# MLP blocks of 512 and 384 tokens in place of 448, in an attention and mixing kernel on one core

## The chip, the cores and the metric

The kernel runs on one core of a Trainium2 chip. The metric is the device time of one execution in microseconds. Before the change it is 916.15 us, the median of three runs (915.28 to 916.17). The profiled execution is a fourth one, 912.93 us long.

## What is computed

Batch 4, 12 heads of 64, so 768 features; 448 tokens per batch. Three stages follow each other:

```python
scores = cap * tanh((q @ k.T / 8) / cap)          # attention, per head
x = softmax(scores) @ v                           # -> (4, 448, 768)
theta = x @ w_theta                               # first mixer
y = w_tok_r @ (x * cos(theta)) + w_tok_i @ (x * sin(theta))
u = x + y
x = u + relu(u @ w_ch)
u = x + (relu(x.T @ w_tok1) @ w_tok2).T           # second mixer, over tokens
out = u + relu(u @ w_ch1) @ w_ch2                 # MLP, 768 -> 1536 -> 768
```

The last line is the MLP. It mixes features only, so any cut of the 4 x 448 tokens into blocks gives the same result.

## The kernel before

Everything is kept transposed: features on the 128 partitions, in six tiles (`D_TILES`), tokens along the free dimension. Each product of two fp32 matrices is made of three fp32r matmuls (`products`, lines 1036 to 1038): high part by high part, high by low, low by high. So every operand is split into a `hi` part (a copy that rounds, mostly on ScalarE) and a `lo` part (value minus `hi`, mostly on VectorE).

Memory: `x_t` holds the activations of all four batches, batch after batch, 6 x 448 floats of each partition per batch. The attention writes it pair of heads by pair, the first mixer adds to it, the token mixer writes it again, and the MLP adds its result in place.

Order of the work after the attention: the angles and token products of the first mixer for four batches, written out; then `token_mix(b)` for four batches; then the MLP, `rise_and_fall(b)` on TensorE. Each engine has its own program, the order in it is as written, and semaphores tie the engines together. `loop_peeled` writes the first and the last batch out and makes a hardware loop of the two in the middle: on TensorE for both stages, on ScalarE and VectorE for `token_mix`.

The MLP of one batch: `up(b, c)` multiplies one of 12 tiles of `w_ch1` by `u` (6 feature tiles x 3 products = 18 matmuls of 448 columns) into PSUM bank 0 or 1; ScalarE makes `relu_hi` of it (L757) and VectorE `relu_lo` (L1020); `down(b, c)` multiplies the tile of `w_ch2` by these (6 output tiles x 3 products = 18 matmuls) and adds up in the banks 2 to 7 over the 12 tiles. TensorE's order is up(1), down(0), up(2), down(1), ..., up(11), down(10), down(11). So `down(10)` and `down(11)`, 36 matmuls, lie between the last `up` of a batch and the first `up` of the next one. In that time ScalarE makes `relu_hi` of tile 11 and then `u_hi` of the next batch (L742), and VectorE makes `u_lo` of it (L928); `up` of the next batch waits for `u_lo_made`. After that VectorE adds the banks 2 to 7 to `x_t` (L1029), and SyncE stores the result in two halves (L512).

`up(0, 0)` comes early, inside `token_mix(3)`, in the place in which the other batches have `channel(b + 1, 0)`: after `tokens_up(b, 1)`. It too waits for `u_lo_made`.

The activations of batches 2 and 3 are written to memory before the MLP (`spill`, L492), since the weights of tile 11 and two of the three `relu` buffers lie in their place; they are read back into the place of batches 0 and 1 as soon as the outputs of these are stored (L517).

Of the kernel before, what the change touches and what calls it, by code (L numbers as in the profile page):

```python
# [19 lines left out]
F32 = mybir.dt.float32  # L20
# [7 lines left out]
P = 128  # L28
# [8 lines left out]
BANK = 512  # L37
HEAD_TILES = SEQ // P
# [27 lines left out]
def mixer_kernel(nc, kq_t, v, cap, w_theta, w_tok_r_t, w_tok_i_t, w_ch, w_tok1, w_tok2,  # L66
                 w_ch1, w_ch2, out_t, sum_scratch, inverse_scratch, u_scratch):
    ctx = ExitStack()
    with ctx:
# [14 lines left out]
        x_t = place("x_t", [P, BATCH * D_TILES * SEQ], F32, AT_X)  # L84

        def x_tile(b, d, n=1):

            return x_t[:, bass.ds((b * D_TILES + d) * SEQ, n * SEQ)]
# [104 lines left out]
        o += 21504  # L193
# [24 lines left out]
        ring_at = [o, AT_X + X_BYTES // 2 + 12288, AT_X + X_BYTES // 2 + 12288 + 3584]  # L218
        relu_hi = [place(f"relu_hi{s}", [P, SEQ], F32R, at) for s, at in enumerate(ring_at)]
        relu_lo = [place(f"relu_lo{s}", [P, SEQ], F32R, at + 1792) for s, at in enumerate(ring_at)]  # L220
        assert o + 3584 <= AT_TOP
# [103 lines left out]
        def after(engine, semaphore, value):  # L325

            if not isinstance(value, int) or value > 0:
                engine.wait_ge(semaphore, value)

        def loop_peeled(engine, n, body):  # L330

            body(0)
            with engine.Fori(1, n - 1) as i:
                body(i)
            body(n - 1)

# [32 lines left out]
        def _(sp):  # L371
# [48 lines left out]
            def copy_x(b):  # L420

                after(sp, x_rows_ready, BEFORE[b])
                x_b = x_tile(b, 0, D_TILES).rearrange("p (d n) -> p d n", n=SEQ)
                sp.dma_start(x_batch[:, :, 0:SEQ], x_b).then_inc(x_copied, 16)
                if b % 2 == 0:
                    next_b = x_tile(b + 1, 0, D_TILES).rearrange("p (d n) -> p d n", n=SEQ)
# [61 lines left out]

            def spill(b):

                sp.wait_ge(u2_made, D_TILES * (b + 1))
                sp.dma_start(u_scratch[b - 2].rearrange("(d p) n -> p d n", p=P),  # L492
                             x_t[:, b * D_TILES * SEQ:(b + 1) * D_TILES * SEQ].rearrange(
                                 "p (d n) -> p d n", n=SEQ)).then_inc(spilled, 16)
# [13 lines left out]
            for b in range(BATCH):  # L508
                for half in range(2):
                    d0 = 3 * half  # L510
                    sp.wait_ge(out_made, D_TILES * b + d0 + 3)
                    sp.dma_start(out_t[b, d0 * P:(d0 + 3) * P, :].rearrange("(d p) n -> p d n", p=P),  # L512
                                 x_t[:, ((b % 2) * D_TILES + d0) * SEQ:((b % 2) * D_TILES + d0 + 3) * SEQ
                                     ].rearrange("p (d n) -> p d n", n=SEQ)).then_inc(out_stored, 16)
# [841 lines left out]
```

## Time and profile before

| | |
|---|---|
| profiled execution | 912.93 us |
| its span, first to last instruction | 910.9 us |
| TensorE busy | 893.6 us, 98% of the span |
| VectorE, ScalarE, GpSimd busy | 438.4, 305.9, 191.0 us |
| mean DMA rate | 62 GB/s |
| stages: attention; first mixer; token mix; MLP | 0 to 182; 182 to 387; 387 to 553; 546 to 911 us |

The busy time of TensorE is that of overlapping matmuls, whose ends are modelled: 368 ns are given for one of 448 columns, though the next starts 207 ns later. The distance from start to start is what a matmul costs. `PE` is TensorE, `PEld` its weight loads, `DVE` VectorE, `ACT` ScalarE, `SP` SyncE. In the chain of waits matmuls of the MLP alone (lines 1036 to 1038) are the largest part.

### The profile page before, as it was taken

The numbers are of one execution on the slowest core, as the hardware profiler recorded it, in microseconds if no ns is written. First come the engines' busy times: TensorE is split into PE (matmuls) and PEld (weight loads), VectorE is DVE, ScalarE is ACT, GpSimd is POOL, SyncE is SP. The second block draws the span as 40 slices with busy tenths as digits, with TensorE's granted clock in tenths as the row PEclk, the third lists the DMA queues.
The fourth block names the chain that finished last, engine by engine and source line by source line (L and its number), as shares of the span: only waits on it lengthen the run. The fifth ranks groups of instructions, "written<-read, shape, count | busy, mean of one in ns | idle before, by whom it ended". The sixth has DMA issues, their size and how long they took to land.

```text
span 910.9 us, 12549 instructions
## 1 busy us (share of the span) xinstructions
PE 893.6 (98%) x5248; PEld 754.9 (83%) x5248; DVE 438.4 (48%) x593; ACT 305.9 (34%) x355; POOL 191.0 (21%) x139
## 2 busy tenths in 40 slices
PE   8999999998999999999999999999999999999998
PEld 5445444597999889999999999999999999999997
DVE  5899998798584968724243442223200310031002
ACT  6999998645151434412122121112000100010000
POOL 0245545247050533270000024600000000000000
PEclk9999999999999999999999999999999999999999
DMA  6555764412020200230000136200300030000001
GB/s 160 163 135 150 181 171 114 124 43 61 1 70 1 62 1 27 78 110 1 1 0 0 61 104 217 87 1 1 122 1 0 1 121 0 0 25 37 1 1 61
DMA packets 40514, 56.76 MB, mean 62 GB/s; under 512 B 5744, under 2 KB 36624, under 8 KB 40464
## 3 DMA queue, kind: packets, MB, share of 16 engines
q1 hardware_dynamic: 40240, 55.82, 21.0%
q8 instruction: 37, 0.61, 0.3%
q10 hardware_dynamic: 224, 0.23, 0.1%
q14 instruction: 13, 0.11, 0.0%
HBM read 41.62 MB, written 8.52 MB: 55 GB/s over the span
## 4 chain that ended last, share of the span: by engine, by line
PE 87%; DVE 8%; issue 2%; ACT 1%; POOL 1%; DMA 0%; DVEq 0%; ACTq 0%
PE psum L1036 23%; PE psum L1038 23%; PE psum L1037 23%; PE psum L1078 8%; PE psum L1048 5%; PE psum L1053 2%; PE psum L1105 2%; DVE sin_z L897 2%; PE psum L1201 1%; DVE reduced L890 1%; DVE reduced L886 1%; DVE tile_sums L790 1%; PE psum L1151 1%; DVE tail_z L914 0%; DMA kq_raw<-kq_t 0%
## 5 line engine op out<-in xcount | busy, mean ns | idle before, releaser
L1020 DVE SCALAR_TENSOR_TENSOR relu_lo<-psum,relu_hi 128x448 fp32r<-128x448 f32 x48 | 30.0, 625 | 280.5 <-PE psum L1038 263.6
L757 ACT ACTIVATE relu_hi<-psum 128x448 fp32r<-128x448 f32 x48 | 26.2, 546 | 312.7 <-PE psum L1038 303.0
L1037 PE MATMUL psum<-relu_lo,mlp 128*128 128x448 f32 x288 | 106.1, 368 | 0.0
L1038 PE MATMUL psum<-relu_hi,mlp 128*128 128x448 f32 x288 | 106.1, 368 | 0.0
L1038 PE MATMUL psum<-u_hi,mlp 128*128 128x448 f32 x288 | 106.1, 368 | 0.0
L1036 PE MATMUL psum<-relu_hi,mlp 128*128 128x448 f32 x288 | 106.1, 368 | 0.0
L1037 PE MATMUL psum<-u_lo,mlp 128*128 128x448 f32 x288 | 106.1, 368 | 0.0
L1036 PE MATMUL psum<-u_hi,mlp 128*128 128x448 f32 x288 | 106.0, 368 | 0.0
L1078 PE MATMUL psum<-ring,values 128*32 128x448 f32 x768 | 82.5, 549 | 1.2 <-issue 1.2
L631 ACT ACTIVATE ring<-psum,score_scale 128x1792 f32<-128x1792 f32 (+1 forms) x48 | 75.3, 1568 | 17.9 <-PE psum L1105 10.0
L634 ACT ACTIVATE ring<-ring,cap_col 128x1792 f32<-128x1792 f32 (+1 forms) x48 | 77.1, 1606 | 1.6
L1078 PEld LDWEIGHTS psum<-ring,values 128*32 128x32 f32 x768 | 23.1, 111 | 45.3 <-issue 45.1
L1036 PE MATMUL psum<-theta_hi,x_hi 128*128 128x384 f32 x168 | 58.7, 349 | 0.0
L1036 PEld LDWEIGHTS psum<-relu_hi,mlp 128*128 128x128 f32 x288 | 54.1, 188 | 5.4
L1038 PEld LDWEIGHTS psum<-relu_hi,mlp 128*128 128x128 f32 x288 | 54.1, 188 | 5.4
L1037 PEld LDWEIGHTS psum<-relu_lo,mlp 128*128 128x128 f32 x288 | 54.1, 188 | 5.4
L1036 PEld LDWEIGHTS psum<-u_hi,mlp 128*128 128x128 f32 x288 | 54.1, 188 | 5.4
L1038 PEld LDWEIGHTS psum<-u_hi,mlp 128*128 128x128 f32 x288 | 54.1, 188 | 5.4
L1037 PEld LDWEIGHTS psum<-u_lo,mlp 128*128 128x128 f32 x288 | 54.1, 188 | 5.3
L1037 PE MATMUL psum<-theta_lo,x_hi 128*128 128x384 f32 x168 | 56.5, 336 | 0.0
L1038 PE MATMUL psum<-theta_hi,x_lo 128*128 128x384 f32 x168 | 56.5, 336 | 0.0
L1036 PE MATMUL psum<-u_hi,channel_hi 128*128 128x448 f32 x144 | 54.1, 375 | 0.0
(134 smaller groups left out, 1971.7 us busy)
## 6 DMA issues: line engine op xcount, KB each, us to landing
kq_raw<-kq_t SPq DMA_DIRECT2D x47, 224.0 KB, 3.8
mlp_raw<-moe_w_ch SPq DMA_DIRECT2D x24, 384.0 KB, 6.6
values<-v SPq DMA_DIRECT2D x48, 112.0 KB, 3.4
inverse_rows<-inverse_scratch SPq DMA_DIRECT2D x12, 448.0 KB, 6.0
x_batch<-x_t SPq DMA_DIRECT2D x4, 1344.0 KB, 6.4
out_t<-x_t SPq DMA_DIRECT2D x8, 672.0 KB, 3.1
u_scratch<-x_t SPq DMA_DIRECT2D x2, 1344.0 KB, 5.3
x_t<-u_scratch SPq DMA_DIRECT2D x2, 1344.0 KB, 5.8
```

The lines of the kernel that those rows point to most:

```text
L631: act.activation(places, psum[:, first:end, 0:SEQ], ACT.Tanh, scale=score_scale[:, :]).then_inc(tanh_done, 1)
L634: act.activation(places, places, ACT.Exp, scale=cap_col[:, :]).then_inc(probs_ready, 1)
L757: act.activation(relu_hi[c % 3][:, :], psum[:, c % 2, 0:SEQ], ACT.Relu).then_inc(relu_hi_made, 1)
L897: dve.tensor_scalar(sin_z[slot_of(b, m)][:, :], reduced[:, :], PI_BELOW, -PI_BELOW, ALU.min, ALU.max).then_inc(angles_ready, 1)
L1020: dve.scalar_tensor_tensor(out=relu_lo[c % 3][:, :], in0=psum[:, c % 2, 0:SEQ], scalar=0.0, in1=relu_hi[c % 3][:, :].bitcast(F32), op0=ALU ...
L1036: pe.matmul(out, left[0], right[0], start=start, stop=False)
L1037: pe.matmul(out, left[0], right[1], start=False, stop=False)
L1038: return pe.matmul(out, left[1], right[0], start=False, stop=stop)
L1048: b_mm = pe.matmul(psum[:, b_tile, 0:SEQ], left[s][b_rows, b_keys], right[s][b_rows, queries], start=step == 0, stop=step == 2 and b_tile ...
L1053: a_mm = pe.matmul(psum[:, a_tile, 0:SEQ], left[s][a_rows, a_keys], right[s][a_rows, queries], start=step == 0 and a_tile != T, stop=step ...
L1078: mm = pe.matmul(psum[rows, VALUES_BANK, 0:SEQ], own[:, block, 32 * h:32 * h + 32], ring[:, ring_place(pair, tile), :], start=n == 0, stop ...
L1105: mm = pe.matmul(psum[32 * n:32 * n + 32, SUMS_BANK, 0:SEQ], weights[:, :], moving, start=True, stop=True)
```

## The change

- The MLP goes over four blocks of tokens, `BLOCKS`: tokens 0 to 512 and 512 to 896 of batches 0 and 1 taken together, and the same of batches 2 and 3. Block 0 holds batch 0 and 64 tokens of batch 1.
- `x_t` is laid out as [half of two batches, feature tile, 896 tokens], so that a block is one strided view of it. A batch is now six rows of 448 with 896 between their starts.
- `u_hi` and `u_lo` of the MLP become `wide_hi` and `wide_lo`, with 512 places per feature tile; the `relu` buffers get 512 places. What lies behind them moves up by 3,072 bytes.
- A block's output is stored per half of the features and per batch: four DMAs for a block of 512 (448 and 64 tokens, twice), two for one of 384.
- The loops over batches are written out on all engines.

The diff, cut:

```diff
+BLOCKS = ((0, BANK), (BANK, 2 * SEQ)) * 2
...
-        x_t = place("x_t", [P, BATCH * D_TILES * SEQ], F32, AT_X)
+        x_t = place("x_t", [P, 2, D_TILES, 2 * SEQ], F32, AT_X)
+        def x_tile(b, d):
+            return x_t[:, b // 2, d, b % 2 * SEQ:(b % 2 + 1) * SEQ]
+        def x_of(b):
+            return x_t[:, b // 2, :, b % 2 * SEQ:(b % 2 + 1) * SEQ]
+        def x_block(k):
+            first, end = BLOCKS[k]
+            return x_t[:, 0, :, first:end]
...
-        o += 21504
+        wide_hi = place("wide_hi", [P, D_TILES, BANK], F32R, o)
+        wide_lo = place("wide_lo", [P, D_TILES, BANK], F32R, o + 12288)
+        o += 24576
...
+            for k, (first, end) in enumerate(BLOCKS):
                 for half in range(2):
                     d0 = 3 * half
+                    sp.wait_ge(out_made, D_TILES * k + d0 + 3)
+                    for b in range(2):
+                        n0, n1 = max(first, b * SEQ), min(end, (b + 1) * SEQ)
+                        if n0 < n1:
+                            sp.dma_start(out_t[k // 2 * 2 + b, d0 * P:(d0 + 3) * P, n0 - b * SEQ:n1 - b * SEQ
...
+                if k < 2:
+                    sp.wait_ge(out_stored, stored)
+                    sp.dma_start(x_block(k), spilled_rows[:, :, first:end]).then_inc(u_reloaded[k], 16)
...
-                if isinstance(b, int) and b == BATCH - 1:
-                    act.wait_ge(u2_made, D_TILES)
-                    make_u_hi(0)
+                if b == BATCH - 1:
+                    act.wait_ge(u2_made, D_TILES * 2)
+                    make_wide_hi(0)
...
-                    act.activation(relu_hi[c % 3][:, :], psum[:, c % 2, 0:SEQ], ACT.Relu
+                    act.activation(relu_hi[c % 3][:, 0:n_tokens], psum[:, c % 2, 0:n_tokens], ACT.Relu
...
+            def make_wide_lo(k):
+                tokens = slice(0, BLOCKS[k][1] - BLOCKS[k][0])
+                dve.wait_ge(u_hi_made, BATCH + k + 1)
+                dve.tensor_tensor(wide_lo[:, :, tokens], x_block(k), wide_hi[:, :, tokens].bitcast(F32),
+                                  ALU.subtract).then_inc(u_lo_made, 1)
...
-                    mm = products(psum[:, c % 2, 0:SEQ], (mlp[c][:, 0, part], mlp[c][:, 1, part]),
-                                  (u_hi[:, k, :], u_lo[:, k, :]), k == 0, k == D_TILES - 1)
+                    mm = products(psum[:, c % 2, tokens], (mlp[c][:, 0, part], mlp[c][:, 1, part]),
+                                  (wide_hi[:, d, tokens], wide_lo[:, d, tokens]), d == 0, d == D_TILES - 1)
...
-            loop_peeled(pe, BATCH, rise_and_fall)
+            for k in range(len(BLOCKS)):
+                rise_and_fall(k)
```

The order of the instructions stays the same outside the loops; what changes is their size, block by block. On ScalarE, from the last `relu_hi` of the second batch of the MLP to the third (before; the number behind a name is that of the buffer):

```order
L757 ACTIVATE relu_hi_151<-psum 128x448
L757 ACTIVATE relu_hi_152<-psum 128x448
L742 ACTIVATE u_hi<-x_t 128x2688
L757 ACTIVATE relu_hi_150<-psum 128x448
L757 ACTIVATE relu_hi_151<-psum 128x448
```

The same place now, between the second block and the third:

```order
L761 ACTIVATE relu_hi_153<-psum 128x384
L761 ACTIVATE relu_hi_154<-psum 128x384
L697 ACTIVATE wide_hi<-x_t 128x3072
L761 ACTIVATE relu_hi_152<-psum 128x512
L761 ACTIVATE relu_hi_153<-psum 128x512
```

The copy between the blocks has 3,072 elements per partition instead of 2,688, and it stands behind a block of 384 columns. On VectorE, the end of `token_mix(3)` before (`u_lo` is what `up(0, 0)` waits for, the first and third row add the token mixer's result):

```order
L982 TENSOR_TENSOR x_t<-psum,block_t 128x448
L928 TENSOR_TENSOR u_lo<-x_t,u_hi 128x2688
L982 TENSOR_TENSOR x_t<-psum,block_t 128x448
L976 SCALAR_TENSOR_TENSOR hidden_lo<-psum,hidden_hi 128x384 x2
L982 TENSOR_TENSOR x_t<-psum,block_t 128x448 x3
L1020 SCALAR_TENSOR_TENSOR relu_lo_153<-psum,relu_hi_150 128x448
```

And now:

```order
L990 TENSOR_TENSOR x_t<-psum,block_t 128x448
L936 TENSOR_TENSOR wide_lo<-x_t,wide_hi 128x3072
L990 TENSOR_TENSOR x_t<-psum,block_t 128x448
L984 SCALAR_TENSOR_TENSOR hidden_lo<-psum,hidden_hi 128x384 x2
L990 TENSOR_TENSOR x_t<-psum,block_t 128x448 x3
L1032 SCALAR_TENSOR_TENSOR relu_lo_155<-psum,relu_hi_152 128x512
```

Nothing moved there but the size of the subtraction, 2,688 to 3,072.

## Rows read from the trace of the kernel before

**Rows 1.** The page: busy time and share of the span of each engine.

```profile
PE 893.6 (98%) x5248; PEld 754.9 (83%) x5248; DVE 438.4 (48%) x593; ACT 305.9 (34%) x355; POOL 191.0 (21%) x139
```

**Rows 2.** Stretches, TensorE: length, busy (matmuls), granted clock, DMA share, GB/s.

```profile
638.80:728.06 89.26, 89.26 (x434) 1.00 0.09 31
728.06:817.32 89.26, 89.26 (x434) 1.00 0.09 31
240.74:243.69 2.95, 2.95 (x19) 1.00 0.00 0
262.15:266.42 4.27, 4.27 (x22) 1.00 0.60 164
```

**Rows 3.** Timeline, TensorE, token mix: start us, length us, line, tiles, shape.

```profile
419.63 0.34 PE L1036 MATMUL psum<-rows_hi,tok_hi 112*128 112x384 f32 x1
423.88 0.37 PE L1036 MATMUL psum<-u_hi,channel_hi 128*128 128x448 f32 x1
464.56 0.37 PE L1036 MATMUL psum<-u_hi,channel_hi 128*128 128x448 f32 x1
505.25 0.37 PE L1036 MATMUL psum<-u_hi,channel_hi 128*128 128x448 f32 x1
545.94 0.36 PE L1036 MATMUL psum<-u_hi,mlp 128*128 128x448 f32 x1
```

**Rows 4.** Timeline, TensorE, first mixer: angle products (384), token products (448).

```profile
240.91 0.34 PE L1038 MATMUL psum<-theta_hi,x_lo 128*128 128x384 f32 x1
243.51 0.34 PE L1038 MATMUL psum<-theta_hi,x_lo 128*128 128x384 f32 x1
262.15 0.36 PE L1036 MATMUL psum<-token_hi,tail_hi 128*128 128x448 f32 x1
266.42 0.37 PE L1036 MATMUL psum<-token_hi,tail_hi 128*128 128x448 f32 x1
```

**Rows 5.** Timeline around `up(0, 0)`: ScalarE, VectorE, weight loads (PEld).

```profile
539.93 2.44 ACT L691 ACTIVATE u_hi<-x_t 128x2688 fp32r<-128x2688 f32 x1
542.41 3.02 DVE L928 TENSOR_TENSOR u_lo<-x_t,u_hi 128x2688 fp32r<-128x2688 f32 x1 [1.11 <-ACT u_hi L691]
545.76 0.19 PEld L1036 LDWEIGHTS psum<-u_hi,mlp 128*128 128x128 f32 x1
```

**Rows 6.** Timeline between the second and the third batch of the MLP.

```profile
720.82 0.55 ACT L757 ACTIVATE relu_hi<-psum 128x448 fp32r<-128x448 f32 x1 [6.89 <-PE psum L1038]
721.26 2.44 ACT L742 ACTIVATE u_hi<-x_t 128x2688 fp32r<-128x2688 f32 x1
723.73 2.96 DVE L928 TENSOR_TENSOR u_lo<-x_t,u_hi 128x2688 fp32r<-128x2688 f32 x1 [1.71 <-ACT u_hi L742]
727.85 0.19 PEld L1036 LDWEIGHTS psum<-u_hi,mlp 128*128 128x128 f32 x1
```

**Rows 7.** Single lines: durations min/median/max in ns, first and last start.

```profile
L645 ACT ACTIVATE x_hi<-x_t x1: 504/504/504, 270.7 to 270.7; 128x384 fp32r<-128x384 f32 x1
L863 DVE TENSOR_TENSOR x_lo<-x_t,x_hi x2: 553/553/553, 170.1 to 274.3; 128x384 fp32r<-128x384 f32 x2
L859 DVE TENSOR_TENSOR x_lo<-x_t,x_hi x4: 2948/3106/3272, 167.3 to 329.9; 128x2688 fp32r<-128x2688 f32 x4
L1029 DVE TENSOR_TENSOR x_t<-psum,x_t x24: 616/618/626, 637.3 to 906.8; 128x448 f32<-128x448 f32 x24
```

**Rows 8.** The end: chain's last pieces, last matmul; output DMAs of the page.

```profile
903.68 3.72 DVE x_t L1029 x6
906.37 0.37 PE L1038 MATMUL psum<-relu_hi,mlp 128*128 128x448 f32 x1
out_t<-x_t SPq DMA_DIRECT2D x8, 672.0 KB, 3.1
```

More of the change, by code:

```diff
@@ L216, in mixer_kernel @@
         o = AT_EARLY + 2 * 12288
[L218 to L221, printed above, removed]
+        ring_at = [o, AT_X + X_BYTES // 2 + 12288, AT_X + X_BYTES // 2 + 12288 + 4096]
+        relu_hi = [place(f"relu_hi{s}", [P, BANK], F32R, at) for s, at in enumerate(ring_at)]
+        relu_lo = [place(f"relu_lo{s}", [P, BANK], F32R, at + 2048) for s, at in enumerate(ring_at)]
+        assert o + 4096 <= AT_TOP and 12288 + 2 * 4096 <= X_BYTES // 2
         THETA_BANKS = (0, 1, 4, 5)
@@ L1262, in token_mix @@
                 pe.wait_ge(u_lo_made, b + 2)
-                if isinstance(b, int) and b == BATCH - 1:
+                if b == BATCH - 1:
                     up(0, 0)
@@ L1268, in token_mix, with down @@
                     tokens_down(b, d)
-            loop_peeled(pe, BATCH, token_mix)
-            def down(b, c):
-                n = C_TILES * b + c
-                if isinstance(n, int) and n == 0:
+            for b in range(BATCH):
+                token_mix(b)
+            def down(k, c):
+                n = C_TILES * k + c
+                tokens = slice(0, BLOCKS[k][1] - BLOCKS[k][0])
+                if n == 0:
                     pe.wait_ge(u2_made, D_TILES * BATCH)
@@ L1283, in down, with rise_and_fall @@
                     if c == 0:
[L1284 removed]
+                        after(pe, out_made, D_TILES * (k - 1) + d + 1)
                     part = slice(d * P, (d + 1) * P)
[L1286 to L1287 removed]
+                    mm = products(psum[:, 2 + d, tokens], (mlp[c][:, 2, part], mlp[c][:, 3, part]),
+                                  (relu_hi[c % 3][:, tokens], relu_lo[c % 3][:, tokens]),
                                   c == 0, c == C_TILES - 1)
                     mm.then_inc(down_steps, 1)
[L1291 to L1292 removed]
+            def rise_and_fall(k):
+                pe.wait_ge(u_lo_made, BATCH + k + 1)
                 for c in range(C_TILES):
[L1294 to L1295 removed]
+                    if not (k == 0 and c == 0):
+                        up(k, c)
                     if c >= 1:
[L1297 to L1300 removed]
+                        down(k, c - 1)
+                down(k, C_TILES - 1)
+            for k in range(len(BLOCKS)):
+                rise_and_fall(k)
 def _heads_transposed(a):
```

136 lines of the change are left out of this document (59 added, 77 removed).

## The prediction

> **What bounds the kernel now.** I read the page first. TensorE is busy 98% of the span, no other engine half of it [rows 1]. But busy time of overlapping matmuls can't show a gap of 0.1 us, so the second view is the timeline of TensorE, for the distances from start to start. Between the first `up` of the second batch of the MLP and the first `up` of the third lie 24 groups of 18 = 432 matmuls in 89.26 us, and as many in the same time up to the fourth batch [rows 2]: 206.6 ns for one, at the full granted clock of 1.00, with no gap. Four batches are 1,728 matmuls, 357.0 us, 39% of the profiled execution. Nothing but TensorE's own rate bounds that stage. So three questions decide the change: what a matmul of 512 and one of 384 columns cost where one of 448 costs 206.6 ns; whether a wait opens where none is; whether the loops cost anything.
>
> **Term 1: the matmuls.** Their number stays: 4 blocks x 24 groups x 18 = 1,728. Now 864 have 512 columns and 864 have 384, in place of 1,728 with 448; the sum of the columns is the same. So I price a pair (one of 512, one of 384) against two of 448, 413.2 ns. A tenth of a nanosecond per pair is 0.09 us.
>
> Rows of 384 columns: the second half of `tokens_up` is 24 matmuls from 419.63 to 423.88, 4.25 us, 177 ns each [rows 3]; the angle products have 15 steps from 240.91 to 243.51, 2.60 us, 173.3 ns [rows 4]. Rows of 448: the MLP at 206.6, and the token products of the first mixer with 21 from 262.15 to 266.42, 4.27 us, 203.3 ns [rows 4]. All at a granted clock of 1.00 [rows 2]; at 2.4 GHz and one column per cycle 384 columns take 160 ns and 448 take 186.7. What lies above that is 13.3 and 17 ns for 384 and 16.7 and 20 ns for 448. So there are two kinds of stream, 3.3 ns apart, and in each kind 64 columns more cost 30 ns (206.6 - 177, and 203.3 - 173.3), not 26.7: the extra grows with the columns.
>
> No row shows 512 columns. Continuing the straight line, 512 cost 206.6 + 30 = 236.6 ns, and 384 in the MLP cost 176.6: a pair 413.2 ns, a gain of nothing. If instead the extra is a fixed amount per matmul, 20 ns at 448, then 512 cost 233.3 and 384 cost 180: again 413.3. Any law that is a constant plus a rate gives zero, whatever its numbers, since neither the count nor the columns change. Only a bend between 384 and 512 gives something. The bounds: from below 512 columns at the bare clock, 213.3 ns, with 384 at the cheapest row, 173.3: 386.6 ns a pair, 864 x 26.6 ns = 23 us less. From above, 512 at the straight line plus two steps of the size by which the two kinds of stream differ, 236.6 + 6.6, with 384 at 180: 423.2 ns, 8.6 us more. I take zero, since two independent pairs of rows show the same slope.
>
> The Trainium skill's "TensorE: Matmul & The Clock Gate", section "Back-to-back issue gap", gives a matmul at full clock its columns at 2.4 GHz plus about 2.5 ns. The trace does not agree here, the extra is 17 to 20 ns at 448 columns and differs at 384. By that rule, as a fixed charge, the change would be worth nothing as well; if the MLP's blocks of 512 alone came down to the 215.7 ns that the page gives for 512, the sum would be 18 us less.
>
> **Term 2: the copies in front of `up(0, 0)`.** It stands behind `tokens_up(3, 1)` and waits for the low parts. Now ScalarE starts the copy at 539.93 and VectorE subtracts from 542.41 to 545.43; the weight load of `up(0, 0)` starts at 545.76 [rows 5]: 0.33 us of slack. After the change both have 3,072 elements. From a single 384-element and a 2,688-element instruction of the same kinds I get a rate: ScalarE (2.44 - 0.504) / 2,304 = 0.84 ns per element, VectorE (2.96 - 0.553) / 2,304 = 1.04 ns [rows 5, 6, 7]. So 384 more cost 0.32 and 0.40 us, the low parts come 0.72 us later, and TensorE waits 0.39 us. The source is now strided; the nearest rows are those of `x_lo`, 2,948 to 3,272 ns for the 2,688 elements of a strided tile against 2,960 [rows 6, 7], so between 0 and 0.3 us may come on top. I take 0.4 us (0.3 to 0.8). Behind this wait on TensorE stand `up(0, 0)` and `tokens_down(3, 3)` to `(3, 5)`, and all engines wait for those. ScalarE's new wait for the twelfth `u2_made` in place of the sixth costs nothing: batch 1 was through the token mixer long before.
>
> For the other three batches the copy keeps its 2,688 elements with a strided source; with 0.3 us slack each it costs 0 (at most 0.1 each).
>
> **Term 3: the wait between the second and the third block.** Before, `relu_hi` of tile 11 starts at 720.82, the low parts are done at 723.73 + 2.96 = 726.69, 5.87 us later, and the next weight load comes at 727.85, 7.03 us after 720.82 [rows 6]: a slack of 1.16 us, covered by `down(10)` and `down(11)`, 36 matmuls. Between blocks 1 and 2 these 36 have only 384 columns: the cover shrinks by 36 x 30 ns = 1.08 us to 5.95 us. The copies are for a block of 512: plus 0.72 us, less 0.05 us for the shorter `relu_hi`, 6.54 us. TensorE waits 0.59 us; with the stride up to 0.3 more. I take 0.6 us. At the two other borders it is the other way round, cover 8.1 us and copies 5.2 us: nothing. The read-back of block 2 is issued some 80 us before, so it doesn't show.
>
> **Term 4: the loops.** The hardware loop on TensorE runs `rise_and_fall(1)` from 638.80 to 728.06, jumps back, and runs `(2)` to 817.32: 89.26 us both, and 432 x 206.6 ns fills that [rows 2]. In the token mixer the steps from batch to batch are 40.68 (423.88 to 464.56), 40.69 and 40.69 us, one of them with the jump back [rows 3]. So the jumps cost nothing, and writing the loops out brings nothing. On the other engines they lie beside TensorE's work.
>
> The Trainium skill's "Runtime: NRT & Kernel Launch", section "Instruction fetch mechanics", says that a taken branch breaks the sequential prefetch and makes a stall. The steps of [rows 2, 3] don't show one on TensorE. By that rule the change would save the stalls of the jumps, by the rows 0.
>
> **Term 5: the end.** The last block has 384 columns. VectorE's last addition, behind the last matmul (906.37) and ending at 903.68 + 3.72 = 907.40 [rows 8], shrinks from 618 ns by 64 elements x 1.04 ns, 0.07 us. The store behind it takes 3.1 us for 672 KB [rows 8]; now it is 576 KB in one DMA. By bytes alone it saves up to 0.44 us, by a fixed time nothing; I take 0.1. In all -0.2 us (-0.5 to 0). The additional small stores of 64 tokens belong to blocks 0 and 2, with a block of 384 columns behind them that takes 432 x 177 ns = 76 us.
>
> **Sum.** 0 + 0.4 + 0.6 + 0 - 0.2 = +0.8 us on the profiled 912.93: 913.7 us. The median of the timed runs is 3.2 us above the profiled execution, so the forecast is 916.15 + 0.8 = 917.0 us, no change that can be told: a measurement of this kernel tells about 0.2%, 1.8 us, from nothing. Its own range is 916 to 918.5 us.
>
> **Rivals.**
>
> *The pair gets cheaper (chance 0.28).* A bend downwards: some of the 20 ns extra doesn't grow up to 512 columns. For it: the two kinds of stream show that the extra isn't a matter of the columns alone, and the new tiles start at other places (rows of 2,048 bytes in place of 1,792), so the MLP may fall into the cheaper kind. Against it: the slope is 30 ns in both kinds. One step of 3.3 ns on one of the two sizes is 2.9 us: 914.1 us. One on both, the cheaper kind throughout, is 5.7 us: 911.2. Without any extra at 512, the lower bound, 894.
>
> *The pair gets dearer (chance 0.24 with the next point).* The place is each of the 864 matmuls of 512 columns, which now fill their PSUM bank to its last column and read the moving tile over its full 2,048 bytes; one step of 3.3 ns on them is 2.9 us more, 919.9 us; two are 922.7. It decides from a pair of 414.4 ns on, where 864 x 1.2 ns and the 0.8 us of the waits pass 1.8 us. Against it: nothing changes between 384 and 448. To the same side go waits of terms 2 and 3 that are 1 us longer than I take them.
>
> *A block border stalls on every block.* If `relu_lo` of 512 columns (about 0.69 us instead of 0.62) reached TensorE's way, each of 48 groups would lose; but between `up(c)` and `down(c)` lie 18 matmuls, 3.7 us, against 1.2 us. I give it 0.01, inside the last chance.
>
> *The change doesn't do what it says.* If a matmul of 512 columns were issued in pieces, the count would rise; the program has it as one instruction, so no chance.
>
> **How the numbers follow.** Forecast 0.48, cheaper 0.28, dearer 0.24. Nearly all of the forecast's case lies within 0.2%, a little of it above; of the cheaper case, the single step (2.0 us less in all) is just outside, so part of it counts as same. That makes faster 0.27, same 0.49, slower 0.24. The range reaches two steps down, a bit below 911.2, and one up: 910.5 to 920.5.
>
> **What would show it.** In the profile after: the distance of starts in blocks of 512 (236.6 ns expected) and of 384 (176.6 or so); the time from the first `up` of block 1 to that of block 2 (76.3 us plus the wait) and of block 0 to 1 (102.2 us for 432); one wait of some 0.4 us before the first matmul of `up(0, 0)` and one of 0.6 us before the first of the third block, both released by VectorE's `wide_lo`; everything up to the end of the first mixer as before. The forecast is wrong if a pair differs from 413.2 ns by over 1.2 ns, or if one of the waits passes 1.5 us.

## The result, and the profile after

The changed kernel takes 907.74 us (median of four runs, 907.54 to 908.40); the kernel before took 915.71 us in the four runs beside it. The ratio is 0.9915, with an interval of 0.9898 to 0.9932: 8.0 us less between the medians, where I had forecast no change, and 907.74 lies below my range of 910.5 to 920.5. The profiled execution after is 907.67 us with a span of 905.6; before they were 912.93 and 910.9.

The page, first line, answers to [rows 1]: TensorE has still 5,248 matmuls, but 5.3 us less of busy time.

```profile
PE 888.3 (98%) x5248; PEld 746.3 (82%) x5248; DVE 438.0 (48%) x593; ACT 305.4 (34%) x355; POOL 189.0 (21%) x139
```

Next the stretches of TensorE in the MLP, which answer to [rows 2]. Columns: window, length and busy time, (instructions that touch it, one or two more than start in it), granted clock, DMA share, GB/s. The windows run from one group's first matmul to another's; the first two lie in block 0 (512 columns), the other two in block 1 (384).

```profile
571.95:597.15 25.20, 25.20 (x110) 1.00 0.20 71
622.02:650.58 28.56, 28.56 (x128) 1.00 0.00 1
669.45:688.53 19.08, 19.08 (x109) 1.00 0.00 1
698.02:719.86 21.84, 21.84 (x128) 1.00 0.00 1
```

They hold 6, 7, 6 and 7 groups of 18 matmuls. So a matmul of 512 columns takes 25.20 / 108 = 233.3 ns in the first and 28.56 / 126 = 226.7 in the second; one of 384 takes 19.08 / 108 = 176.7 and 21.84 / 126 = 173.3. The clock is 1.00 in all four and none has a gap. One size has two rates within a block. The groups with the dear rate are `up` and `down` of tiles 2 to 6 of the weights, those with the cheap one are tiles 7 to 11 (and 0 and 1, apart from the first groups of a block; a cheap group next to a dear one is up to 2.2 ns dearer). Before, 448 columns took 206.6 ns in all tiles [rows 2], with one exception, the very first `up`. Windows of `up(0, 0)` and `up(0, 1)` in the kernel before, 18 matmuls each:

```profile
545.94:549.59 3.65, 3.65 (x20) 1.00 0.05 18
553.27:556.98 3.71, 3.71 (x20) 1.00 0.54 206
```

That is 202.8 ns and 206.1 ns. Both weight tiles, 0 and 1, start 256 bytes beyond a multiple of 512.

From first to last matmul the MLP takes 353.81 us (547.53 to 901.34) in place of 360.43, 6.6 us less. Ahead of it the profiled execution after is 1.6 us later. 0.2 of that is the wait of term 2, on TensorE's matmuls. 0.9 lies in the first mixer (209.38 us in place of 208.51) and 0.5 in the attention (178.86 in place of 178.34), where the granted clock differs: in the same view the kernel after has two stretches at half clock (1.2 GHz), from 146.1 and from 211.0 us, 3.4 us each,

```profile
0.00:20.00 20.00, 16.25 (x121) 1.00 0.75 173
142.00:150.00 8.00, 5.94 (x44) 0.79 0.29 73
208.00:216.00 8.00, 5.45 (x21) 0.79 0.47 143
```

and the kernel before has one, in its first 20 us, in the attention.

```profile
0.00:20.00 20.00, 15.51 (x108) 0.91 0.74 173
142.00:150.00 8.00, 6.40 (x60) 1.00 0.19 52
208.00:216.00 8.00, 5.61 (x28) 1.00 0.57 171
```

Where such a stretch falls, and how many there are, differs from run to run (the mean clock of the timed runs is 0.993 to 0.995 after); what sets one off, no run here shows. So the 0.9 us go with a stretch that the first mixer has only after; with one there the unrolled kernel of the first experiment takes 209.27 us for this stage, in the old layout. The 0.5 us of the attention aren't accounted for: each kernel has one stretch there, and without any this stage took 177.83 us in the first experiment below and 176.58 in another. The new layout, which the attention and the first mixer use too, isn't behind it: with it and blocks of 448 (second experiment) the MLP starts at 546.34 us, before at 545.94. After the last matmul 4.3 us are left instead of 4.6. So the profiled executions differ by +1.6 - 6.6 - 0.3 = -5.3 us, 912.93 to 907.67. The medians differ by more because the profiled execution before was a quick one, 2.8 us below its median; the medians carry the result.

The two new waits are there. Timeline (start us, length us, engine, line, tiles, shapes, [idle before <- releaser]) of the two copies and the first weight load of `up(0, 0)`, answering to [rows 5]:

```profile
541.32 2.77 ACT L697 ACTIVATE wide_hi<-x_t 128x3072 fp32r<-128x3072 f32 x1
...
544.12 3.36 DVE L936 TENSOR_TENSOR wide_lo<-x_t,wide_hi 128x3072 fp32r<-128x3072 f32 x1 [1.44 <-ACT wide_hi L697]
...
547.52 0.19 PEld L1049 LDWEIGHTS psum<-wide_hi,mlp 128*128 128x128 f32 x1 [0.37 <-DVE wide_lo L936]
```

And between blocks 1 and 2, answering to [rows 6]:

```profile
720.06 0.49 ACT L761 ACTIVATE relu_hi<-psum 128x384 fp32r<-128x384 f32 x1 [5.75 <-PE psum L1051]
...
720.44 2.77 ACT L697 ACTIVATE wide_hi<-x_t 128x3072 fp32r<-128x3072 f32 x1
...
723.24 3.36 DVE L936 TENSOR_TENSOR wide_lo<-x_t,wide_hi 128x3072 fp32r<-128x3072 f32 x1 [2.10 <-ACT wide_hi L697]
...
726.65 0.19 PEld L1049 LDWEIGHTS psum<-wide_hi,mlp 128*128 128x128 f32 x1 [0.71 <-DVE wide_lo L936]
```

The bracket of the last row of each says what the weight load waited for: `wide_lo`, 0.37 and 0.71 us. The matmuls themselves lose less, 0.21 and 0.55 us from start to start, since the load before had a lead. The end, answering to [rows 8]:

```profile
901.34 0.34 PE L1051 MATMUL psum<-relu_hi,mlp 128*128 128x384 f32 x1
```

```profile
899.11 3.16 DVE L1042 TENSOR_TENSOR x_t<-psum,x_t 128x384 f32<-128x384 f32 x6 [2.56 <-PE psum L1051]
```

### The profile page after: what moved, and what is told of

Read it like the earlier page. It is cut to its first block, busy times and chain, and to the rows that moved or that the text cites. A ratio compares the mean times of both kernels' runs of the same rounds, so it can differ in the third digit from the quotient of the medians.

```text
span 905.6 us, 12431 instructions
## 1 busy us (share of the span) xinstructions
PE 888.3 (98%) x5248; PEld 746.3 (82%) x5248; DVE 438.0 (48%) x593; ACT 305.4 (34%) x355; POOL 189.0 (21%) x139
## 4 chain that ended last, share of the span: by engine, by line
PE 88%; DVE 7%; issue 2%; ACT 1%; DMA 0%; POOL 0%; DVEq 0%; ACTq 0%
PE psum L1049 23%; PE psum L1050 23%; PE psum L1051 23%; PE psum L1091 8%; PE psum L1061 5%; PE psum L1066 2%; PE psum L1118 2%; DVE sin_z L899 1%; PE psum L1214 1%; DVE reduced L892 1%; DVE reduced L888 1%; DVE wide_lo L936 1%; ACT wide_hi L697 1%; PE psum L1164 1%; DMA kq_raw<-kq_t 0%
## 5 line engine op out<-in xcount | busy, mean ns | idle before, releaser
L1032 DVE SCALAR_TENSOR_TENSOR relu_lo<-psum,relu_hi 128x512 fp32r<-128x512 f32 (+1 forms) x48 | 30.0, 624 | 275.1 <-ACT relu_hi L761 217.3
L761 ACT ACTIVATE relu_hi<-psum 128x512 fp32r<-128x512 f32 (+1 forms) x48 | 26.2, 545 | 307.8 <-PE psum L1051 298.1
L1049 PE MATMUL psum<-wide_hi,mlp 128*128 128x512 f32 (+1 forms) x288 | 105.0, 365 | 0.4 <-DVE wide_lo L936 0.4
L1051 PE MATMUL psum<-wide_hi,mlp 128*128 128x512 f32 (+1 forms) x288 | 104.9, 364 | 0.0
L1051 PE MATMUL psum<-relu_hi,mlp 128*128 128x512 f32 (+1 forms) x288 | 104.8, 364 | 0.0
L1049 PE MATMUL psum<-relu_hi,mlp 128*128 128x512 f32 (+1 forms) x288 | 104.8, 364 | 0.0
L1050 PE MATMUL psum<-wide_lo,mlp 128*128 128x512 f32 (+1 forms) x288 | 104.8, 364 | 0.0
L1050 PE MATMUL psum<-relu_lo,mlp 128*128 128x512 f32 (+1 forms) x288 | 104.7, 364 | 0.0
L1049 PEld LDWEIGHTS psum<-wide_hi,mlp 128*128 128x128 f32 x288 | 54.0, 188 | 7.0 <-DVE wide_lo L936 1.1
L1051 PEld LDWEIGHTS psum<-wide_hi,mlp 128*128 128x128 f32 x288 | 54.0, 188 | 6.1
L1050 PEld LDWEIGHTS psum<-wide_lo,mlp 128*128 128x128 f32 x288 | 54.0, 188 | 6.1
```

What stands on the lines that cost most here:

```text
L761: act.activation(relu_hi[c % 3][:, 0:n_tokens], psum[:, c % 2, 0:n_tokens], ACT.Relu).then_inc(relu_hi_made, 1)
L1032: dve.scalar_tensor_tensor(out=relu_lo[c % 3][:, 0:n_tokens], in0=psum[:, c % 2, 0:n_tokens], scalar=0.0, in1=relu_hi[c % 3][:, 0:n_tokens ...
L1049: pe.matmul(out, left[0], right[0], start=start, stop=False)
L1050: pe.matmul(out, left[0], right[1], start=False, stop=False)
L1051: return pe.matmul(out, left[1], right[0], start=False, stop=stop)
```

## The experiments

The times of the kernel before belong to the same chip as the experiment's.

**Loops written out, nothing else.** The kernel before, with `loop_peeled` unrolled.

```diff
-            body(0)
-            with engine.Fori(1, n - 1) as i:
+            for i in range(n):
```

> The kernel before, with its loops over batches written out and nothing else. Theory R (the gain of 8 us is in the rate of the matmuls, from the blocks and their layout): 0 us, ratio 1.000 within 0.001, 206.6 ns per matmul of the MLP as before. Rival U (the jumps of the hardware loops cost something the distances of the starts don't show): 2 to 8 us less.

Measured: 913.40 us against 913.61, ratio 1.0002 (0.9988 to 1.0016). The second batch of the MLP takes, without the loop, the same 89.26 us as in [rows 2]:

```profile
639.05:728.31 89.26, 89.26 (x434) 1.00 0.09 32
```

The loops cost nothing and the jumps aren't the gain.

**The new layout and code with blocks of 448.** All of the change except the sizes.

```diff
-BLOCKS = ((0, BANK), (BANK, 2 * SEQ)) * 2
+BLOCKS = ((0, SEQ), (SEQ, 2 * SEQ)) * 2
```

> The changed kernel with both blocks of 448 tokens: loops written out, the new layout, rows of 2,048 bytes in wide_hi, wide_lo and relu, but 448 columns in every matmul. Theory L (448 is itself a dear length, 512 and 384 are cheap ones): 206.6 ns per matmul in all 12 weight tiles, 915 to 916 us. Theory G (dear are moving rows that start at an odd multiple of 256 bytes, as every second row of 1,792 bytes does; in the wide tiles all rows start on one grid of 512 bytes): 448 columns fall to 186.7 + 13.3 = 200 ns in the weight tiles 0, 1 and 7 to 11 and to about 203.3 in 2 to 6, so 1,728 x 5.3 ns = 9 us less, about 906.5 us, as good as the changed kernel or a little better, since both waits for the copies go.

Measured: 913.95 us, ratio 1.0003 (0.9990 to 1.0016). Five groups of tiles 2 to 6, and the eight up to the next block, of tiles 7 to 11:

```profile
575.97:594.57 18.60, 18.60 (x91) 1.00 0.00 1
609.44:639.20 29.76, 29.76 (x146) 1.00 0.00 1
```

18.60 / 90 and 29.76 / 144 are both 206.7 ns. So neither the layout nor the new places of `u` are worth anything; the lengths 512 and 384 are the whole gain, in a kernel whose `AT_TOP` lies where it does. And the tiles that are dear at 512 don't stand out at 448: there, all are dear.

**The weights on another start address.** What sets tiles 2 to 6 apart is their place. `AT_TOP` is 167,392, 32 bytes off a grid of 64 bytes; tiles 0, 1 and 7 to 11 start at other constants, all on that grid. The kernel after, with `AT_TOP` 224 bytes lower:

```diff
-AT_TOP = BASE + 150848 + 32
+AT_TOP = BASE + 150848 - 192
```

> The changed kernel with AT_TOP 224 bytes lower, so that what starts there (weights of the two mixers and MLP weight tiles 2 to 6) lies on the same grid of 512 bytes as everything else (before it was 32 bytes off any grid of 64). Theory W (a weight tile off the grid makes its matmuls dear: 233.3 ns against 226.7 at 512 columns, 176.7 against 173.3 at 384): tiles 2 to 6 fall to 226.7 and 173.3, 360 x 6.7 + 360 x 3.3 ns = 3.6 us less in the MLP, tokens_up falls from 176.7 to 173.3 (192 matmuls, 0.6 us); the token products of the first mixer, whose moving operand moves too, may rise from 203.4 to 206.7 (504 matmuls, 1.7 us). In all 904 to 906 us. Rival T (the tiles 2 to 6 are dear for their time in the kernel, by GpSimd's and the DMAs' traffic, or for their number): 233.3 and 176.7 stay, 907.7 us.

Measured: 903.06 us, ratio 0.9890 (0.9868 to 0.9912). The same four kinds of stretch as above (6, 7, 6, 7 groups):

```profile
571.34:595.82 24.48, 24.48 (x109) 1.00 0.21 72
620.30:648.86 28.56, 28.56 (x127) 1.00 0.00 1
667.61:686.33 18.72, 18.72 (x110) 1.00 0.01 1
695.69:717.53 21.84, 21.84 (x128) 1.00 0.00 1
```

24.48 / 108 = 226.7 and 18.72 / 108 = 173.3: the dear rates are gone from tiles 2 to 6, and nothing else in the MLP changed. One wait grew, the one before `up(0, 0)`: the first matmul comes 1.8 us late (0.2 in the kernel after). VectorE's copy took 4.86 us in place of 3.36:

```profile
542.04 1.84 POOL L541 TENSOR_TENSOR mlp<-mlp_raw,mlp 128x768 fp32r<-128x768 f32 x1
...
542.23 4.86 DVE L936 TENSOR_TENSOR wide_lo<-x_t,wide_hi 128x3072 fp32r<-128x3072 f32 x1 [1.44 <-ACT wide_hi L697]
...
547.86 1.85 POOL L541 TENSOR_TENSOR mlp<-mlp_raw,mlp 128x768 fp32r<-128x768 f32 x1
```

In the kernel after, the two instructions met in the other order, and it was GpSimd's that took long, 4.97 us; VectorE's kept its 3.36:

```profile
544.20 4.97 POOL L541 TENSOR_TENSOR mlp<-mlp_raw,mlp 128x768 fp32r<-128x768 f32 x1
```

Of the two, the one that comes second waits. So this kernel pays 1.6 us more for its wait than the kernel after, out of what the new place gains.

**The copies in two halves of the features.** `up` waits for three feature tiles first and then for the other three.

```diff
+                for part in (slice(0, 3), slice(3, D_TILES)):
+                    act.activation(wide_hi[:, part, ...], x_block(k)[:, part, :], ACT.Copy)...
...
+                    if c == 0 and d % 3 == 0:
+                        pe.wait_ge(u_lo_made, BATCH + 2 * k + d // 3 + 1)
```

> The changed kernel with the copy wide_hi and the subtraction wide_lo made in two halves of three feature tiles each, the second half of up's matmuls waiting for the second. Theory: the waits of 0.4 us before up(0, 0) and of 0.56 to 0.7 us before the third block go, since the first half is ready 3.6 us after relu_hi and the second 5.4 us after it, against a cover of 5.95: 1.0 us less, 906.7 us. Rival: the waits were covered by something else that comes just behind, 907.7 us.

Measured: 905.51 us, ratio 0.9910 (0.9894 to 0.9926). The wait between the blocks is gone: `down` of the last tile of block 1 goes over into `up` of block 2 without a bracket. Weight loads of TensorE:

```profile
727.09 0.19 PEld L1053 LDWEIGHTS psum<-relu_lo,mlp 128*128 128x128 f32 x1
727.26 0.19 PEld L1054 LDWEIGHTS psum<-relu_hi,mlp 128*128 128x128 f32 x1
727.43 0.19 PEld L1052 LDWEIGHTS psum<-wide_hi,mlp 128*128 128x128 f32 x1
727.61 0.19 PEld L1053 LDWEIGHTS psum<-wide_lo,mlp 128*128 128x128 f32 x1
```

The wait before `up(0, 0)` is gone too. From first to last matmul the MLP takes 353.05 us, 0.8 less than after: 0.55 for the wait that lies inside it, and 0.2 because the first `up` of each block of 512 runs at 227.5 and 228.9 ns per matmul in place of 233.2 and 234.3. The ratio is that of the change itself within the intervals; 1 us can't be told in the times, in the trace it can.

**The grid and the halves together** (both diffs).

> The changed kernel with both: AT_TOP on the grid of 512 bytes (as in the run with the weights on the grid) and the copies in halves. Theory: the two gains are independent and add up, 903.1 less the 1 us of the two waits, about 902 us; in the trace 226.7 and 173.3 ns in all weight tiles and no wait before the third block. Rival: the stall between the blocks is followed by a quicker stream, so that taking it away gives nothing: 903 us.

Measured: 901.34 us (898.49 to 902.35), ratio 0.9843 (0.9819 to 0.9867). The MLP takes 349.2 us, 11.2 less than before. The wait of 1.8 us ahead of it is gone as well: the token stage, from the first channel matmul to the first of `up(0, 0)`, takes 157.48 us, with the grid alone it took 159.27.

**The grid alone, in the kernel before.** No blocks, no halves:

```diff
-AT_TOP = BASE + 150848 + 32
+AT_TOP = BASE + 150848 - 192
```

> The kernel before (448 columns, loops kept) with AT_TOP 224 bytes lower alone, on the grid of 512 bytes. Theory L (448 columns are a dear length, whatever the weights' place): the MLP stays at 206.6 ns per matmul, only the stages before it gain (channel and token products, 1 to 3 us): 911 to 914 us, ratio 0.997 to 1.000. Rival A (the place of the weights is enough, the whole gain can be had without blocks): the MLP falls to 200 to 203 ns, 6 to 11 us less, 903 to 908 us.

Measured: 905.59 us, ratio 0.9901 (0.9882 to 0.9920). Seven groups over tiles 2 to 6, six over 7 and higher:

```profile
565.45:590.98 25.53, 25.53 (x128) 1.00 0.27 94
612.87:634.76 21.89, 21.89 (x110) 1.00 0.00 1
```

25.53 / 126 = 202.6 and 21.89 / 108 = 202.7 ns. The MLP takes 353.65 us, 6.8 less, and the token stage, whose weights start at `AT_TOP` as well, 157.48 in place of 159.08, 1.6 less. One number gives as much as the whole change.

In the first mixer `AT_TOP` holds the moving operand, and the weights, which are activations, didn't move. So this run varies the moving operand's start by itself. Token products of the second and of the last batch (five and four groups of 21 matmuls):

```profile
261.16:282.44 21.28, 21.28 (x106) 1.00 0.12 33
365.00:382.36 17.36, 17.36 (x85) 1.00 0.17 64
```

21.28 / 105 = 202.7 ns, where it was 203.3 before, and 17.36 / 84 = 206.7, where it was 204.5 (17.18 / 84). The stage as a whole takes 209.20 us, with the loops written out and nothing else 209.27. So the dear 206.7 can also come up with everything on the grid, weights and moving operand; in the run with the grid under the kernel after it does so in the same products.

**Other lengths on the grid** (the kernel after with `AT_TOP` 224 lower and these `BLOCKS`). Batches 0 and 1 are cut at 480, 2 and 3 at 464:

```diff
+BLOCKS = ((0, 480), (480, 2 * SEQ), (0, 464), (464, 2 * SEQ))
```

> The changed kernel with AT_TOP on the grid and four lengths in one kernel: the blocks of batches 0 and 1 are 480 and 416 tokens, those of 2 and 3 are 464 and 432. Theory M (cheap are whole multiples of 128 columns, all others carry 20 ns): 220.0, 193.3, 213.3 and 200.0 ns. Theory S (the extra is 13.3 ns unless the length is 448): 213.3, 186.7, 206.7 and 193.3. Theory E (a length is dear by a rule on 64 columns, odd multiples of 64 dear and everything between in between): 216.7, 190.0 and the like.

Measured in a single run: 907.64 us. Stretches in the blocks of 480 and 416 columns (17 and 20 groups):

```profile
571.01:637.31 66.30, 66.30 (x307) 1.00 0.09 31
651.90:719.70 67.80, 67.80 (x362) 1.00 0.07 23
```

66.30 / 306 = 216.7 ns and 67.80 / 360 = 188.3; the other two are 208.9 (464) and 195.9 (432). And cut at 504 and 496:

```diff
+BLOCKS = ((0, 504), (504, 2 * SEQ), (0, 496), (496, 2 * SEQ))
```

> As the run before, with lengths of 504 and 392 tokens (batches 0 and 1) and 496 and 400 (batches 2 and 3). Theory M (whole multiples of 128 columns cheap, all others 20 ns above the bare columns): 230.0, 183.3, 226.7 and 186.7 ns. Theory S (13.3 ns above the bare columns at every length but 448): 223.3, 176.7, 220.0 and 180.0 ns.

Measured in a single run: 909.09 us. Stretches of 504 and 392 columns (19 and 20 groups):

```profile
565.91:643.43 77.52, 77.52 (x343) 1.00 0.18 62
657.98:721.82 63.84, 63.84 (x362) 1.00 0.07 25
```

77.52 / 342 = 226.7 ns, as much as 512 columns take, and 63.84 / 360 = 177.3. With 496 at 223.3 and 400 at 180.0, what a matmul of the MLP on the grid costs above its columns at 2.4 GHz is (448 from the kernel before on the grid, 512 and 384 from the kernel after on it):

| columns | 384 | 392 | 400 | 416 | 432 | 448 | 464 | 480 | 496 | 504 | 512 |
|---|---|---|---|---|---|---|---|---|---|---|---|
| ns above | 13.3 | 14.0 | 13.3 | 15.0 | 15.9 | 16.0 | 15.6 | 16.7 | 16.7 | 16.7 | 13.3 |
| ns with its partner to 896 | 400.0 | 404.0 | 403.3 | 405.0 | 404.8 | 405.3 | 404.8 | 405.0 | 403.3 | 404.0 | 400.0 |

512 with 384 is the best pair, by 5.3 ns over two of 448: 864 x 5.3 ns = 4.6 us. Every other cut is within 2 ns of 448. From 384 to 504 the extra rises from 13.3 to 16.7 ns, not evenly; the last 8 columns to 512 cost nothing, and that makes the pair.

**A grid of 64 bytes, and no larger one.** The first move put `AT_TOP` at 256 modulo 512, like the other tiles. Now the kernel after with `AT_TOP` 32 bytes lower, at 0 modulo 64 and 64 modulo 128:

```diff
-AT_TOP = BASE + 150848 + 32
+AT_TOP = BASE + 150848
```

> The changed kernel with AT_TOP 32 bytes lower, on a grid of 64 bytes but not of 128, 256 or 512. Theory 64 (a weight tile has to start at a multiple of 64 bytes): 226.7 and 173.3 ns in all 12 weight tiles, as with AT_TOP at 224 bytes lower, 903 us. Rival 512 (the weight tiles have to lie like the moving rows in a grid of 128 to 512 bytes): tiles 2 to 6 stay at 233.3 and 176.7 ns, 907 us.

Measured in a single run: 900.33 us. Tiles 2 to 6 (five groups), then 7 and higher (seven):

```profile
571.47:592.07 20.60, 20.60 (x91) 1.00 0.04 14
616.67:645.23 28.56, 28.56 (x127) 1.00 0.00 1
```

20.60 / 90 = 228.9 ns, 28.56 / 126 = 226.7: on this grid most of the 6.7 ns are back, not all (at 384 columns all of the 3.3 are: 173.3). The MLP takes 350.95 us, 1.0 more than with the first move (349.96), and the kernel is quicker all the same, since the stages ahead gain: the token stage takes 156.36 us in place of 159.27. In it a channel product that nothing interrupts runs at 200.0 ns in place of 202.6, and VectorE's copy began 0.05 us ahead of GpSimd's instruction and kept its 3.36 us, so that `up(0, 0)` came 0.3 us late and not 1.8.

**Only the MLP off the grid, at 448.** The kernel before with `AT_TOP` on the grid, but tiles 2 to 6 of the MLP 32 bytes off it; the token mixer's buffers, which share the place, 64 bytes higher.

```diff
-AT_TOP = BASE + 150848 + 32
+AT_TOP = BASE + 150848 - 192
-        tok1_hi = place("tok1_hi", ..., AT_TOP + 36864)
+        tok1_hi = place("tok1_hi", ..., AT_TOP + 36928)
...
-        tile_at = (... + [AT_TOP + 12288 * j for j in range(5)]
+        tile_at = (... + [AT_TOP + 32 + 12288 * j for j in range(5)]
```

> The kernel before with AT_TOP on the grid of 512 bytes, but the MLP weight tiles 2 to 6 moved 32 bytes off it (the buffers of the token mixer's weights, which would overlap tile 4, move by 64 bytes). Theory K (with 448 columns the dear rate, once entered, is kept): the MLP starts at 202.7 ns in tiles 0 and 1, goes to 206.7 at tile 2 and stays there to the end of the kernel, in tiles 7 to 11 and in the next batches' 0 and 1 as well. Rival P (each tile has the rate of its own place): 206.7 only in tiles 2 to 6, 202.7 in 0, 1 and 7 to 11 of all four batches.

Measured in a single run: 908.34 us. Tiles 2 to 6 (six groups), 7 and higher (seven):

```profile
568.76:590.84 22.08, 22.08 (x109) 1.00 0.33 113
612.83:638.36 25.53, 25.53 (x127) 1.00 0.00 1
```

22.08 / 108 = 204.4 ns off the grid and 25.53 / 126 = 202.6 on it, batch after batch: here 448 behaves as 512 does, but the dear rate is 204.4, not 206.7. The place isn't that of the kernel before either: the tiles start 288 bytes beyond a multiple of 512, in the kernel before 480.

**Only the MLP on the grid, at 448.** The kernel before (`AT_TOP` unchanged, 32 off), tiles 2 to 6 at `AT_TOP + 32`, token buffers 64 higher.

```diff
+        tile_at = (... + [AT_TOP + 32 + 12288 * j for j in range(5)]
```

> The kernel before with all as it was, AT_TOP 32 bytes off, but the MLP weight tiles 2 to 6 32 bytes higher, which puts them on the grid, so that all 12 lie on it (the buffers of the token mixer's weights move by 64 bytes, still 32 off). Theory K (the dear rate is kept once entered, whatever the later tiles): what the stage before leaves goes on: 206.7 ns through the whole MLP if the channel and token matmuls before it leave it, or 202.7 throughout, but no change of rate with the tile. Rival P (each tile has the rate of its own place): 202.7 in all tiles, 6.9 us less than before. A change at tile 2 would speak against both.

Measured in a single run: 909.30 us. Tiles 2 to 6, five groups:

```profile
574.61:592.85 18.24, 18.24 (x91) 1.00 0.16 56
```

18.24 / 90 = 202.7 ns, and so everywhere else in the MLP: 353.7 us, 6.7 less than before.

**Only the token buffers, 64 bytes higher,** still 32 off the grid; the MLP's tiles untouched.

```diff
+        tok1_hi = place("tok1_hi", ..., AT_TOP + 36928)
```

> The kernel before with only the buffers of the token mixer's weights 64 bytes higher (still 32 bytes off the grid of 64), the MLP weight tiles 2 to 6 off the grid as before. Theory H (the stage ahead of the MLP sets the pattern in which its stream runs, and moving these buffers was what changed it): tiles 0, 1 and 7 to 11 at 202.7, tiles 2 to 6 at 204.4 ns, as in the run with the tiles alone off the grid; about 4 to 5 us less than before. Rival T (the place of the MLP tiles does it): 206.7 in all tiles, as before.

Measured in a single run: 911.48 us. Two groups with tiles 0 and 1, five with tiles 2 to 6, seven after those:

```profile
551.96:559.25 7.29, 7.29 (x37) 1.00 0.78 240
574.12:592.72 18.60, 18.60 (x91) 1.00 0.00 1
611.31:637.35 26.04, 26.04 (x128) 1.00 0.00 1
```

7.29 / 36 = 202.5 ns, 18.60 / 90 = 206.7, 26.04 / 126 = 206.7. The cheap rate lasts until the first matmul of tile 2, the first of the MLP off the grid. Then the dear one stays, over the tiles 7 to 11 on the grid, and over tiles 0 and 1 of the next batches, which had run at 202.5. In the kernel before it began one tile earlier, in `up(0, 1)`, ahead of any tile off the grid; the move of the token buffers alone put that off.

Those buffers show more. The second half of `tokens_up` is 24 matmuls of 384 columns, whose weights are `tok1_hi` and `tok1_lo`. They lie 32 bytes off the grid in both kernels, at 480 beyond a multiple of 512 before and at 32 now, and take 4.16 us in place of 4.25 [rows 3]:

```profile
418.71:422.87 4.16, 4.16 (x25) 1.00 0.00 0
```

4.16 / 24 = 173.3 ns in place of 177, less than on the grid (4.19 us, 174.6 ns, in the kernel before with `AT_TOP` 224 lower). So a place off the grid isn't always dear.

**Only tiles 2 to 6, 32 bytes lower,** on the grid of 64 at another residue (448 modulo 512).

```diff
+        tile_at = (... + [AT_TOP - 32 + 12288 * j for j in range(5)]
```

> The kernel before with only the MLP weight tiles 2 to 6 moved, 32 bytes lower and so on a grid of 64 bytes; the token mixer's buffers as before. Theory H (the stage ahead sets the pattern): 206.7 ns in all 12 tiles, as before, although all lie on the grid. Rival T (the place of the MLP tiles does it): 202.7 ns in all 12, 6.8 us less than before.

Measured in a single run: 912.37 us. Tiles 2 to 6 (six groups), then 7 and higher (seven):

```profile
575.71:597.31 21.60, 21.60 (x110) 1.00 0.14 50
615.67:641.71 26.04, 26.04 (x127) 1.00 0.00 1
```

21.60 / 108 = 200.0 ns, and 26.04 / 126 = 206.7. The tiles moved are the cheapest of all at 448, the ones untouched as dear as ever, though they lie on the grid too: they are dear from `up(0, 1)` on, as in the kernel before. Neither theory had this.

**The best version.** The kernel after with `AT_TOP` 32 lower and the copies in halves.

> The changed kernel with AT_TOP 32 bytes lower (grid of 64) and the copies in halves. Theory: as the run with the grid of 512 and the halves, 901.3 us, within 1 us, ratio to before 0.984 to 0.987. Rival (the grid of 64 is better than that of 512 in the stages before the MLP): 899 to 900 us, ratio 0.982.

Measured: 900.93 us (898.77 to 902.02), ratio 0.9849 (0.9832 to 0.9866). Against the other place of the weights, 901.34 us with 0.9843, no difference can be told. Both beat the change (0.9915) and the kernel before.

## Why the prediction was wrong

**Term 1 is the step that failed.** It said 413.2 ns for a pair and "any law that is a constant plus a rate gives zero", and took zero "since two independent pairs of rows show the same slope". The conclusion from the law is right; the law isn't. The pair costs 233.3 + 176.7 = 410.0 ns in tiles 2 to 6 and 226.7 + 173.3 = 400.0 in the other seven, on average 404.2. That is 9.1 ns under two of 448, and 864 x 9.1 ns = 7.9 us. The MLP shows 6.6 less: 0.6 us goes to the wait of term 3, 0.5 lies where a block or a rate begins (the first `up` takes 233.2 ns per matmul and not 226.7, `down(1)` 228.9), and 0.2 in the first groups of the kernel before, which ran below 206.7.

Two assumptions stood in it. One was the line itself, drawn through 384 and 448 in each of two kinds of stream: it gives 236.6 and 233.3 ns at 512, measured are 233.3 and 226.7, so 512 lies 3.3 and 6.6 ns below it, and on the grid the lengths between don't lie on a line either (table above). The other was that the MLP keeps one kind. I had not asked what divides the kinds. (The clock of 1.00 in `tokens_up`, for which I had named [rows 2], stands in none of them; the trace has it.) In `tokens_up` [rows 3], at the dear rate, the stationary weights lie at `AT_TOP`, off the grid; in the two products of [rows 4], at the cheap one, `AT_TOP` holds the moving operand and the weights are activations. The MLP has both sorts of places in its 12 tiles, and in the kernel before ran them at 206.7, all but the first `up`, which hid it. But 3.3 ns between streams of one shape at one clock stood in the rows, and it says that something other than the columns sets the rate. I had written that among the rivals: "the MLP may fall into the cheaper kind", at 911.2 us with one step on both sizes. That there was a step down was right. The reason I gave, the new places of the wide tiles, wasn't: with these and 448 columns nothing fell (second experiment). And it was short in size for the 512: in tiles 7 to 11 they are 236.6 - 226.7 = 9.9 ns below what I expected, three steps, and the 384 one step.

How much of that is the place and how much the length? In tiles 7 to 11, 448 runs at 206.7 and 512 with 384 at 400.0, so the change brings 13.3 ns a pair there, but with all weights on the grid two of 448 cost 405.3. So the length is worth 5.3 ns of it (4.6 us over 864 pairs; the MLPs on the grid differ by 353.65 - 349.96 = 3.7 us, with the wait of 0.6 in the second), and the other 8.0 ns are the dear rate of 448. The change doesn't take the weights off their bad place; it makes TensorE leave the dear rate at tile 7, at once. At 448 and in this kernel it doesn't leave it at all (the kernel with the new layout and 448, and the one with moved token buffers). The kernel before on the grid, 6.8 us faster in its MLP without any blocks, is the proof that most of this was to be had otherwise.

The Trainium skill's "TensorE: Matmul & The Clock Gate", section "Back-to-back issue gap", gives the 2.5 ns above the columns as the gap of an isolated matmul, about 216 ns at 512, which the prediction left out, and 131 ns at 512 for a stream of weight loads and matmuls. The trace agrees with neither: 226.7 ns at best, 13.3 to 16.7 above the columns on the grid. As a fixed charge the 2.5 ns would have made 512 and 384 worth nothing.

**Term 2** (0.4 us): 0.37 on the weight load, 0.21 on the matmuls, which is what the kernel pays; the wait was right, its price half of mine. The copies took 2.77 and 3.36 us where the rates per element gave 2.76 and 3.36; the strided source cost nothing that shows.

**Term 3** (0.6 us, from a cover of 36 shorter matmuls): right. 36 matmuls of `down(10)` and `down(11)` span 6.79 us instead of 6.24, 0.55 more. That the cover shrinks on the same border on which the copies grow is what made the wait; the halved copies removed it, as expected.

**Term 4** (0): right, shown by the loops alone (1.0002) and by the layout at 448 (1.0003). The stall that the Trainium skill's "Runtime: NRT & Kernel Launch", section "Instruction fetch mechanics", gives a taken branch whose target isn't in the window of pages that were fetched isn't seen here: 89.26 us with and without the jump. Whether the target lay in that window, no run shows.

**Term 5** (-0.2 us): right, -0.3.

**The rivals.** "The pair gets cheaper", with a chance of 0.28, is what happened. "The pair gets dearer" was wrong: filling the PSUM bank to its last column costs nothing, and 512 is the cheapest length per column of all that were run. No stall on the groups appeared. The chances of same (0.49) against faster (0.27) were set by the straight line, and its bounds, worked out at 386.6 to 423.2 ns a pair, did hold the measured 404.2; I cut the range to two steps down although 894 was my own lower end.

**What stays open.** Why a rate belongs to a place of the weights, and why at 448 it can begin ahead of the tiles off the grid and outlast them, no run shows. 448 columns ran at 200.0, 202.7, 204.4 and 206.7 ns here, by the places and by what ran before. That a place 32 bytes off the 64-byte grid is dear is shown at 512 and 384 by two other places of the same weights, and at 448 by 204.4 against 202.6 ns in one kernel, and by the whole MLP at 202.7 once tiles 2 to 6 were moved on top of the token buffers. But only two places off the grid were tried in the MLP, 480 and, at 448 columns alone, 288 beyond a multiple of 512. That the rate is set by the residue modulo 64 alone is refuted by 228.9 against 226.7 at 512, by 200.0 against 206.7 at 448, and by the 173.3 ns of `tokens_up` off the grid. The start of the moving operand was varied by itself in the first mixer alone (203.3 to 202.7 in one batch, 204.5 to 206.7 in another), not in the MLP, and blocks of 512 and 384 in the channel stage were not tried.

## What to carry to other kernels

When a stage is nothing but back-to-back matmuls, divide a gapless stretch by its count for every operand tile, and compare tiles of one shape at one clock: 3 ns between them is 1.5% of the stage and has a cause, here the start address of the weights for a good part. Don't put a line through rates of streams with different operands; try one length and one place at a time. Before a stage is recut, try its weights at another start address, on a 64-byte grid first: here one constant gave 0.9901, the recut 0.9915, both with the copies halved 0.9843.

## What the hardware showed that I had not expected

- A start address of the weights 32 bytes off a grid of 64 bytes cost TensorE's stream in the MLP: 233.3 against 226.7 ns at 512 columns, 176.7 against 173.3 at 384, 204.4 or 206.7 against 202.7 at 448. It isn't so at every such place: `tokens_up` ran at 173.3 ns at 32 beyond a multiple of 512, and at 177 at 480. The weight load's own duration doesn't show it, 188 ns in every kernel; the distance does.
- 504 columns take as long as 512, 226.7 ns, and 392 longer by 4.0 ns than 384, where 8 columns at 2.4 GHz are 3.3 ns.
- At 448 a dear rate, once entered, can last to the end of the kernel, some 340 us, over tiles that ran cheaper before. It also came up with all operands on the grid (206.7 ns, token products of the last batch).
- VectorE's subtraction of 3,072 elements takes 3.36 us, but 4.86 where GpSimd's tensor operation began 0.19 us before it; in the other order it is GpSimd's that goes from 1.84 to 4.97 us, and 544.20 + 4.97 is 1.69 us after VectorE's end. The Trainium skill's "SBUF — State Buffer", section "SBUF: two separate sides", has the pair of ports that the two share as a lock for whole instructions, not a split of the bandwidth; the trace agrees: what is left of the later one behind the end of the earlier, 1.69 us, is near its own 1.84. A shift of 2 us upstream swaps which of the two is late, and one of them is on TensorE's path.
